# A wkv recurrence and two feed-forward blocks on one core: bonus 3 in a dense PSUM bank, and six instructions at other places in their engines' order

## What is computed

```python
for t in range(S):                                  # attention, a decayed recurrence
    cur = einsum('bhd,bhe->bhde', u[None] * kt, vt)
    y[:, :, t] = einsum('bhd,bhde->bhe', rt, state + cur)
    state = wt[:, :, :, None] * state + einsum('bhd,bhe->bhde', kt, vt)
# first block, x_prev is x one step earlier
xk, xr = mu_k * x + (1 - mu_k) * x_prev, mu_r * x + (1 - mu_r) * x_prev
x = sigmoid(xr @ w_r) * (maximum(xk @ w_k, 0) ** 2 @ w_v)
# second block
h = gelu(x @ w_in); u, v = h[..., :512], h[..., 512:]
v_n = (v - mean(v)) / sqrt(var(v) + 1e-6) * g_ln
out = x + (u * (einsum('ts,bsd->btd', w_sg, v_n) + b_sg[None, :, None])) @ w_out
```

## Time and profile before

| | |
|---|---|
| median of 3 runs | 331.51 us (331.38 to 332.08) |
| the profiled execution's own time | 331.37 us |
| its span | 329.5 us |
| granted TensorE clock, mean | 1.0 of full speed |
| PE busy | 318.6 us, 97% |
| PEld busy | 299.1 us, 91% |
| DVE busy | 199.8 us, 61% |
| ACT busy | 151.3 us, 46% |
| POOL busy | 97.4 us, 30% |

### The profile page before, as it was taken

How to read it: one execution, slowest core, us unless ns; L and a number is a source line. 1 busy time by engine, 2 the same in 40 slices (tenths; PEclk the granted TensorE clock), 3 DMA queues, 4 the chain that set the end, 5 groups by cost and what they waited for, 6 DMA issues and landing times.

```text
span 329.5 us, 6841 instructions
## 1 busy us (share of the span) xinstructions
PE 318.6 (97%) x2682; PEld 299.1 (91%) x2682; DVE 199.8 (61%) x336; ACT 151.3 (46%) x304; POOL 97.4 (30%) x92
## 2 busy tenths in 40 slices
PE   6989989999999999999999999999999999999996
PEld 2768979888999999999999999899999989999996
DVE  4879895989697398549317065991643546122432
ACT  5477825553455455455546692745113025311100
POOL 5530140273014211430132140772323018313220
PEclk9999999999999999999999999999999999999999
DMA  7996044004504400400006046000000210000012
GB/s 232 408 390 243 0 168 169 0 4 165 169 2 165 166 4 9 163 6 2 8 21 227 0 148 232 7 0 0 2 0 3 95 48 2 0 0 2 0 48 97
DMA packets 11029, 28.08 MB, mean 85 GB/s; under 512 B 1200, under 2 KB 5744, under 8 KB 9712
## 3 DMA queue, kind: packets, MB, share of 16 engines
q1 hardware_dynamic: 10848, 27.46, 23.4%
q10 hardware_dynamic: 144, 0.14, 0.1%
HBM read 24.74 MB, written 2.36 MB: 82 GB/s over the span
## 4 chain that ended last, share of the span: by engine, by line
PE 82%; DVE 9%; ACT 4%; issue 3%; POOL 1%; DMA 1%; ACTq 0%; SPq 0%; DVEq 0%; POOLq 0%
PE dense L320 14%; PE dense L321 14%; PE dense L322 14%; PE ps L321 3%; PE ps L320 3%; PE ps L322 3%; PE ps L653 3%; PE py L734 3%; PE dense L316 2%; PE py L720 2%; PE pkt L680 2%; PE pkt L320 2%; PE pkt L321 2%; PE pkt L322 2%; PE pu L320 2%
## 5 line engine op out<-in xcount | busy, mean ns | idle before, releaser
L573 POOL TENSOR_TENSOR k_l<-sq,k_h 128x512 fp32r<-128x512 f32 x22 | 30.3, 1383 | 62.2 <-ACT sq L1002 62.2
L320 PE MATMUL dense<-xkr_h,wk_h 128*128 128x256 f32 x144 | 41.9, 291 | 0.5 <-DVE wk_l L358 0.5
L320 PE MATMUL dense<-k_h,wv_h 128*128 128x256 f32 x144 | 41.2, 286 | 0.4 <-POOL k_l L573 0.4
L322 PE MATMUL dense<-k_h,wv_l 128*128 128x256 f32 x144 | 40.7, 283 | 0.0
L321 PE MATMUL dense<-k_l,wv_h 128*128 128x256 f32 x144 | 40.7, 283 | 0.0
L321 PE MATMUL dense<-xkr_l,wk_h 128*128 128x256 f32 x144 | 40.7, 283 | 0.0
L322 PE MATMUL dense<-xkr_h,wk_l 128*128 128x256 f32 x144 | 40.7, 282 | 0.0
L564 POOL TENSOR_TENSOR rkp<-inw 128x512 f32<-128x512 f32 x12 | 16.2, 1353 | 79.1 <-DVE r_in L1211 63.6
L633 POOL TENSOR_TENSOR gated_l<-gf,gated_h 128x384 fp32r<-128x384 f32 x16 | 16.4, 1027 | 46.1 <-ACT gated_h L1127 36.1
L320 PEld LDWEIGHTS dense<-xkr_h,wk_h 128*128 128x128 f32 x144 | 27.5, 191 | 1.2 <-issue 0.8
L320 PEld LDWEIGHTS dense<-k_h,wv_h 128*128 128x128 f32 x144 | 27.6, 192 | 0.9 <-issue 0.7
(11 more groups left out here) (253 smaller groups left out, 884.1 us busy)
## 6 DMA issues: line engine op xcount, KB each, us to landing
inw<-in_units SPq DMA_DIRECT2D x10, 1026.5 KB, 5.0
vb<-in_vT SPq DMA_DIRECT2D x12, 256.0 KB, 5.1
wsg_raw<-in_wsgT SPq DMA_DIRECT2D x1, 2304.0 KB, 8.4
out_y<-y_out SPq DMA_DIRECT2D x12, 192.0 KB, 1.9
wk_raw<-in_moe_w_k SPq DMA_DIRECT2D x3, 512.0 KB, 9.6
wv_raw<-in_moe_w_v SPq DMA_DIRECT2D x4, 384.0 KB, 14.1
win_raw<-in_moe_w_in SPq DMA_DIRECT2D x3, 512.0 KB, 4.8
inw<-in_units SPq DMA_DIRECT2D x2, 512.0 KB, 5.6
```

Of the source, the lines that this page charges most:

```text
L320: pe.matmul(o, a_h, b_h, start=first and n == 0, stop=False, skip_group_check=True)
L322: mm = pe.matmul(o, a_l, b_h, start=False, stop=last and n == len(pairs) - 1, skip_group_check=True)
L573: pool.tensor_tensor(k2_l[:, 2 * n:2 * n + 2], sq[:, j % 2].rearrange("p (g t) -> p g t", g=2), k2_h[:, 2 * n:2 * n + 2], ALU.subtract).th ...
```

## The change

- PE: `bonus(3)` writes `pm[2]`, bank 2 of `dense`, and stands ahead of `keys_by_step(3)`. It waits for the fourth k tile of stage 0 to be emptied, no more for ACT's copy of the keys. The first r tile of stage 1, the bank's next user, waits for DVE's `bonus(3)`.
- DVE: `carry_on(2)` stands ahead of `mask(3)`. `value` of stage 0's first v tile stands inside `mix(1)`, behind its third low half; the second `value` stands ahead of `carry_on(3)`.
- ACT: `check(2)` stands ahead of `key_high(0, 3)`. In stage 5 the third block of `w_in` is rounded behind the last `key_high`.
- POOL: `products(5)` stands ahead of all `key_low` of stage 1, `products(6)` ahead of the last of them.

```diff
@@ bonus_bank
-            return [py[:], ps[:, 1]][un] if un < N else pkt[:]
+            return [py[:], ps[:, 1]][un] if un < N else pm[2] if un == 3 else pkt[:]
@@ POOL
             products(4)
-            for n in range(2):
-                key_low(1, n)
             products(5)
-            for n in range(2, KG):
+            for n in range(KG - 1):
                 key_low(1, n)
             products(6)
+            key_low(1, KG - 1)
             products(7)
@@ PE, bonus(un)
                 if un == 1:
                     pe.wait_ge(att_done, 1)
+                elif un == 3:
+                    emptied(pe, ("k", 0, KS[3][1]))
                 elif un:
@@ PE, first_mlp
                 if kind == "r" and xs[0] == 0:
                     weights(pe, "wr")
+                    if s == 1:
+                        pe.wait_ge(bonus_done, 4)
@@ PE, stage 0
                     scores(b)
+                    bonus(b)
                     keys_by_step(b)
-                    outputs(b, s + 1)
+                    flag_of(s + 1)
+                    from_state(b)
+                    add_state(b)
+                    from_chunk(b)
@@ ACT, stage 0
                     keys(a)
+                    check(a)
                     key_high(s, 3)
-                    check(a)
                     check(b)
@@ ACT, stage 5
                     key_high(s, 0)
-                    for n in range(1, KG):
-                        high_weight(parts_of("win")[n - 1])
-                        key_high(s, n)
+                    win = parts_of("win")
+                    high_weight(win[0])
+                    key_high(s, 1)
+                    high_weight(win[1])
+                    key_high(s, 2)
+                    key_high(s, 3)
+                    high_weight(win[2])
@@ DVE, mix(s)
+                    if s == 1 and i == KT:
+                        value(0, *VS[0])
@@ DVE, stage 0
                     output(a)
+                    carry_on(a)
                     mask(b)
-                    carry_on(a)
...
                     mix(s + 1)
+                    value(s, *VS[1])
                     carry_on(b)
-                    for tile in VS:
-                        value(s, *tile)
                     scan(a + 2)
```

## The result

The changed kernel takes 328.12 us (median of 4 runs, 327.77 to 328.24) against 331.53 us of the kernel before in the same comparison (331.38 to 332.08): a ratio of 0.9898, 95% interval 0.9886 to 0.9911. That is 3.4 us or 1.0% faster. The forecast was 328.4 us, range 327.8 to 329.3, faster. The profiled execution took 328.14 us with a span of 326.2 us, 3.3 us less than before; the granted clock was 1.0 of full speed in both.

A forecast was written before the change was run, and what follows sets the result against it. The prediction took PE, busy for 318.6 of 329.5 us, to bound the kernel. Gains of 2.45 us by scores(6) and 0.6 us in stage 5 made 3.05 us, so 328.4 us, range 327.8 to 329.3.

The forecast's parts named there:

- The sum: Whole kernel: 2.45 us by scores(6) plus 0.6 us in stage 5 make 3.05 us, giving 328.4 us.
- Stage 0: Bonus 3, carry 2 and the check: PE's flag starts at about 44.05 in place of 45.24, 1.2 us earlier.
- DVE gains less: DVE up to output(3): only its 0.63 us idle can go, so output 3 and mix(1) come 0.6 us earlier.
- The value in `mix(1)`: First value inside mix(1): PE's stall at the second r tile of stage 1 goes, 0.75 us.
- Stage 1: POOL behind scan 5: scores(6) starts at 78.4 in place of 80.88, 2.45 us earlier in all, with DVE the bound.
- row and rule: state(4) meeting POOL: fixed 1.15 us by the row makes 2.55 us; ending a fixed time behind POOL's instruction makes 2.45.
- Stage 5: Third w_in block last: PE's stall on POOL's last low half in the last v tiles goes, 0.6 us.
- (a): state(4) starts before POOL's third low half and takes 0.43 us: up to 0.3 us more, 328.1; chance 0.17.
- (b): DVE, the new bound, costs more by one more meeting with POOL: 329.3; chance 0.13.
- (c): The last stall, in stage 5, doesn't go or only shifts: 329.0; chance 0.06.
- (d): POOL's low halves slip into scan 6, about 1.1 us per meeting: slower, 331.7 for three, 332.9 for four; chance 0.03.
- (e): The edits don't act, the waits removed not being those that ended last: half the gain, 330.0; chance 0.04.

The follow-up runs named there:

- u2_carry: Changed kernel with mask(3) ahead of carry_on(2) on DVE again, bonus 3 staying in the dense bank; 328.84 us.
- u5_bank: Changed kernel with bonus 3 in bank pkt again, behind keys_by_step(3) and its wait for ACT's copy; carry_on(2) stays ahead of mask(3); 328.57 us.
- after: The changed kernel itself, in its first profile, nothing put back; median 328.12 us.
- u4_win: Changed kernel with the third block of w_in rounded ahead of the last k tile of stage 5 again; 328.77 us.
- u6_check: Changed kernel with check(2) behind key_high(0, 3) on ACT again; 328.16 us (median of 2).
- rep_after: The changed kernel timed again, unaltered, with the last group of runs; 327.94 us.
- rep_bank: Second run of the changed kernel with bonus 3 in bank pkt again, beside the repeated changed kernel; 328.39 us.
- f1_wait: Changed kernel with one wait more: POOL's third low half of stage 1 waits until DVE has made the state of unit 4; 327.84 us.
- u3_value: Changed kernel with both values of stage 0 behind carry_on(3) on DVE again; 329.18 us.

## Why the prediction was right

**The sum.** 3.05 us were forecast on the profiled execution. It came to 3.23 by its own time (331.37 to 328.14) and 3.33 by the span's last instruction, of which 0.17 lie ahead of `scores(3)`, where no edit acts. The edits themselves gave 3.16.

**Stage 0** was put at 1.2 us to the flag and is 1.35 by its clock, 1.18 behind `scores(3)` (45.24 - 41.05 against 43.89 - 40.88). The new wait on POOL's product was put at 0.3 and is 0.24. The state met POOL's first low half and took 1.16 us, as worked out. u2_carry and u5_bank show that neither the bank nor the carry alone does it: without the carry the wait passes on to the flag (1.11 us), and without the bank PE waits 0.88 us for the keys' copy.

**DVE gains less** was right: 0.6 us were forecast, the 0.63 us of idle is gone, and output 3 comes 0.72 earlier behind `scores(3)` (48.07 - 41.05 against 47.18 - 40.88). u2_carry, which gives that idle back, loses 0.75 and not 1.15; as said there, PE's slack at `scores(6)` gives the same number.

**The value in `mix(1)`** was put at 0.75 us on PE; `scores(4)` moved by 1.92 in all, 0.77 beyond `from_chunk(3)`. The new short wait expected at `scores(4)` did not appear as a bracket; the tie itself was real, `r_in(4)` ends at 62.87, 0.10 us ahead of it.

**Stage 1** was put at 2.45 us by `scores(6)` and is 2.54. `state(4)` met the third low half, ended 0.28 us behind it (72.86 and 72.58; 0.29 was the rule taken from the earlier trace rows) and lasted 1.38 us. Here row and rule part, as said ahead: by the fixed 1.15 us of the row it would have ended at 72.63. By the Trainium skill's page "SBUF — State Buffer", section "Who interferes with whom", it is blocked until POOL's instruction is done. The trace agrees with the lock, and so do the others: in all seven profiles in which `state(4)` started inside the third low half (after, u2_carry, u4_win, u5_bank, u6_check, rep_after, rep_bank) it lasted 0.99 to 1.38 us and ended 0.27 to 0.29 us behind it. f1_wait shows that this meeting is what bound `scores(6)`. PE was put 0.3 us ahead of that bound and was 0.39.

**Stage 5** was put at 0.6 us and is 0.62; u4_win gives back 0.60.

**The rivals.** (a), the state missing POOL, did not happen in the changed kernel but in u3_value and by force in f1_wait. (b), (c) and (d) did not happen. A part of (e) is true: the check does nothing.

**What fell** is a reading added after the result, not a step of the prediction: that the bank is worth 0.1 us because DVE bounds `scores(6)`. In rep_after PE arrived only 0.28 us ahead of that bound, about the 0.3 us that the prediction itself had, and without the dense bank it arrives 0.6 us later.

## What to carry to other kernels

When two engines arrive at a meeting point within a few tenths of each other, the gain of one edit depends on the others: undone one by one, the edits here cost 1.56, 0.74, 0.87, 0.60 and about 0.5 us (the last with a longer transfer), 4.3 in all, while together they gave 3.16. Work out both arrivals, not the bracket: what an edit costs PE comes out less the time for which PE would have been held at the meeting anyway, as 1.26 - 0.39 = 0.87 us in u3_value. And an instruction of VectorE that must not be late should not stand where a run of GpSimd work is in flight, if both of its inputs lie in SBUF: here one wait added to GpSimd, 0.65 us long, took 0.95 us off such an instruction.

## What had not been expected of the hardware

The time from DVE's store of output 3 to DVE's copy that waits for its transfer within SBUF, of the same size each time, was 3.92, 4.01, 4.01, 4.03, 4.06, 4.12, 4.15, 4.18, 4.20, 4.21, 4.21, 4.23, 4.39 and 4.54 us in fourteen profiles. Where DVE and POOL were the bound, `scores(6)` followed it: 37.07 and 37.13 us behind `scores(3)` at 4.01 and 4.06, 37.29 at 4.20. What sets it wasn't tried.

The eight matmuls with which PE starts, the same in every kernel, took 6.40 us in the profile of before and 5.09 us in that of the changed kernel. In the second PE then waited 0.32 and 0.42 us for DVE's `r_in` of units 0 and 1, where it had waited for neither before, so that by `scores(3)` 0.17 us were left of the 1.31. What sets their duration wasn't tried.
